# A blocked causal attention and two MLP layers: masks folded into the maximum product, with a copied operand

## What is computed

```python
scores = scale * np.matmul(q, k.transpose(0, 1, 3, 2))
mask = (pos[:, None] // 64) >= (pos[None, :] // 64)
scores = np.where(mask, scores, -1000000000.0)
scores = scores - np.max(scores, axis=-1, keepdims=True)
attn = np.exp(scores)
attn = attn / (np.sum(attn, axis=-1, keepdims=True) + 1e-09)
out = np.matmul(attn, v)
```

## Time and profile before

| | us |
|---|---|
| median of 3 runs | 841.53 (839.37 to 844.37) |
| the profiled execution | 839.87 |
| its span, first to last instruction | 838.0 |
| attention, up to the first MLP product | 236.7 |
| PE busy | 768.6 (92%) |
| DVE busy | 478.2 (57%) |
| ACT busy | 332.3 (40%) |
| POOL busy | 210.2 (25%) |

### The profile page before, as it was taken

How to read it: one execution, slowest core, us unless ns; L and a number is a source line. 1 busy time by engine, 2 the same in 40 slices (tenths; PEclk the granted TensorE clock), 3 DMA queues, 4 the chain that set the end, 5 groups by cost and what they waited for, 6 DMA issues and landing times.

```text
span 838.0 us, 13290 instructions
## 1 busy us (share of the span) xinstructions
PE 768.6 (92%) x4119; PEld 677.7 (81%) x4120; DVE 478.2 (57%) x809; ACT 332.3 (40%) x647; POOL 210.2 (25%) x219
## 2 busy tenths in 40 slices
PE   2989999999999999999999994299999999999993
PEld 1867888788799999999999993278888888888882
DVE  7537777788779484848576456632122483544261
ACT  1435665667563343526161410231211473433250
POOL 5446667666420000000010000212122132122111
PEclk9989999999999999999999997589999999999998
DMA  2665545454210000000100010377110057160000
GB/s 99 227 211 165 142 123 146 141 142 137 66 30 0 1 1 38 1 38 1 39 1 38 1 38 38 124 281 287 38 50 29 25 183 285 38 235 36 14 25 8
DMA packets 50626, 73.79 MB, mean 88 GB/s; under 512 B 28396, under 2 KB 28556, under 8 KB 50576
## 3 DMA queue, kind: packets, MB, share of 16 engines
q1 hardware_dynamic: 46976, 63.71, 23.3%
q0 software_dynamic: 3600, 9.44, 3.1%
HBM read 64.77 MB, written 10.56 MB: 90 GB/s over the span
## 4 chain that ended last, share of the span: by engine, by line
PE 79%; DVE 9%; DMA 5%; SPq 3%; issue 2%; ACT 1%; POOL 1%; POOLq 0%; DVEq 0%
PE ps L687 20%; PE ps L688 19%; PE ps L689 19%; PE ps L640 7%; DMA sums<-o_raw 3%; PE ps L618 3%; PE ps L793 2%; PE ps L677 2%; PE ps L619 2%; PE ps L591 2%; PE ps L766 1%; DVE sig L1126 1%; DMA qk_raw<-qkT 1%; SPq L333 1%; DMA inv_scratch<-sums 1%
## 5 line engine op out<-in xcount | busy, mean ns | idle before, releaser
L640 PE MATMUL ps<-pT,v_sb 128*128 128x320 f32 (+4 forms) x448 | 117.3, 386 | 1.5 <-issue 1.5
L640 PEld LDWEIGHTS ps<-pT,v_sb 128*128 128x128 f32 (+1 forms) x448 | 72.1, 193 | 18.0 <-issue 9.1
L817 ACT ACTIVATE pT<-ps 128x256 f32<-128x256 f32 (+2 forms) x192 | 64.4, 389 | 28.5 <-PE ps L619 25.3
L687 PE MATMUL ps<-we_hi,xgT_hi 128*128 x176 | 72.8, 413 | 2.2 <-DVE xgT_lo L1295 2.2
L687 PE MATMUL ps<-we_hi,hT_hi 128*128 x176 | 71.5, 407 | 2.7 <-DVE hT_lo L1301 2.7
L688 PE MATMUL ps<-we_lo,xgT_hi 128*128 x176 | 70.5, 401 | 0.0
L689 PE MATMUL ps<-we_hi,xgT_lo 128*128 x176 | 70.4, 400 | 0.0
L688 PE MATMUL ps<-we_lo,hT_hi 128*128 x176 | 69.6, 395 | 0.0
L689 PE MATMUL ps<-we_hi,hT_lo 128*128 x176 | 69.6, 395 | 0.0
L687 PE MATMUL ps<-ksq_hi,wm_hi 128*128 128x384 f32 x192 | 65.8, 343 | 1.6 <-DVE yT L1136 1.6
L999 DVE TENSOR_REDUCE negm<-ps 128x1 fp32r<-128x128 f32 (+3 forms) x128 | 57.1, 469 | 15.4 <-PE ps L592 15.1
(11 more groups left out here) (205 smaller groups left out, 1730.1 us busy)
## 6 DMA issues: line engine op xcount, KB each, us to landing
we_raw<-w SPq DMA_DIRECT2D x12, 2048.0 KB, 9.3
qk_raw<-qkT SPq DMA_DIRECT2D x32, 576.0 KB, 4.2
inv<-inv_scratch SPq DMA_DIRECT2D x32, 144.0 KB, 3.0
y_scratch<-ytok SPq DMA_DIRECT2D x6, 768.0 KB, 3.4
v_sb<-v SPq DMA_DIRECT2D x32, 128.0 KB, 3.5
wm_raw<-w_k SPq DMA_DIRECT2D x4, 512.0 KB, 4.5
wm_raw<-w_v SPq DMA_DIRECT2D x4, 512.0 KB, 6.1
wm_raw<-w_r SPq DMA_DIRECT2D x4, 256.0 KB, 4.9
```

The source lines that it names most:

```text
L640: last = mm(ps[:, OUTB + half, q0 - 256 * half:q1 - 256 * half], v_sb[0:rows, j % 2, c, cols], pT[0:rows, i % 2, at + q0:at + q1], start=( ...
L687: mm(dst, a_hi, b_hi, start=(k == 0), stop=False)
L817: return nc.scalar.activation(dst, src, ACT.Exp, **kw)
```

## The change

`q_hi`, `k_both`, `q_lo` and `k_hi` become two tiles a buffer: `hi` (128 rows; q and k) and `aug` (69 rows; three planes, QMAX = 0, QLO = 1, KHI = 2). Rows 0 to 63 of the planes QMAX and KHI are filled by a DMA from `hi` within SBUF (`load_aug`); rows 64 to 68 are written by VectorE once a buffer. The maximum product becomes one product of these 69 rows for each tile, with the mask in rows 65 to 68, and `mask_q` x `mask_k` is gone. For the maximum k's lower half is left out. The subtraction for q goes from GpSimd to VectorE, the cast of q from VectorE to ScalarE, ScalarE's second cast of k is gone. The 1e-9 is added by ScalarE's copy as a bias. Weights come in 20 pieces of 512 columns (256 KB), one a turn in turns 0 to 19. The operands of MLP step 0 are made later: w = 0 in heads 28 to 31 chunk by chunk, w = 1 within step 0, and step 1's w = 1 after step 0's sigmoid. The diff, cut to its core:

```diff
             def load_qk(i):
                 wait(sp, q_split, i - 1)
-                wait(sp, k_is_hi, i - 1)
+                wait(sp, k_split, i - 1)
...
+            def load_aug(i):
+
+                sp.wait_ge(q_is_hi, i + 1)
+                sp.wait_ge(k_is_dup, i + 1)
+                sp.dma_start(aug[i % NBUF][0:DH, QMAX:KHI + 1:KHI - QMAX, 0:S].bitcast(F32),
+                             hi[i % NBUF][0:DH, :, :].bitcast(F32)).then_inc(aug_loaded[i % NBUF], 16)
...
             def load_wm(q):
-                for at, src, n, cols in ((0, wk_in, 1, FF), (WR, wr_in, 1, DM), (WV, wv_in, 2, DM)):
-                    dst = wm_raw[:, at + n * q * cols:at + n * (q + 1) * cols].rearrange("p (c f) -> p c f", c=n)
-                    sp.dma_start(dst, src[:, n * q:n * q + n, :]).then_inc(wmlp_loaded, 16)
...
+                wait(sp, wmlp_loaded[q % WTURN], 16 * (q // WTURN))
+                sp.dma_start(wm_raw[:, q * WLOAD:(q + 1) * WLOAD], src).then_inc(wmlp_loaded[q % WTURN], 16)
...
             load_v(0)
+            load_aug(0)
+            load_aug(1)
             load_qk(2)
             load_row(0)
             load_qk(3)
+            load_aug(2)
...
                 if i % 2 == 0 and i + 2 < NHEAD:
                     load_v(i // 2 + 1)
-                if i < 4:
+                if i < WMLP // WLOAD:
                     load_wm(i)
+                if i + NBUF < NHEAD:
+                    load_aug(i + NBUF)
...
             def head_max(i, groups):
...
-                    pe.wait_ge(q_is_hi, i + 1)
-                    pe.wait_ge(k_split, i + 1)
+                    pe.wait_ge(aug_loaded[i % NBUF], 16 * (i // NBUF) + 16)
...
-                            mm(ps[:, bank, col:col + keys], q_tile, k_both[b][:, 0:keys], start=True, stop=False)
-                            last = mm(ps[:, bank, col + keys - BLK:col + keys], mask_q[:, :], mask_k[:, :],
-                                      start=False, stop=True)
+                            last = mm(ps[:, bank, col:col + keys], q_tile, a[:, KHI, 0:keys], start=True, stop=True)
...
-                        mm(dst, k_both[b][:, keys], q_hi[b][:, q0:q1], start=True, stop=False)
-                        last = mm(dst, k_hi[:, b, keys], q_lo[:, b, q0:q1], start=False, stop=True)
+                        mm(dst, hi[b][:, KEY, keys], hi[b][:, Q, q0:q1], start=True, stop=False)
+                        last = mm(dst, aug[b][:, KHI, keys], aug[b][:, QLO, q0:q1], start=False, stop=True)
...
-                pe.wait_ge(xm_split, 2 * s + 1)
+                if s:
+                    pe.wait_ge(xm_split, 2 * s)
+                else:
+                    pe.wait_ge(xm0_split, DC)
...
-                nc.scalar.activation(o_raw[:, i % NBUF, q0:q1], ps[:, OUTB + half, 0:q1 - q0],
-                                     ACT.Copy).then_inc(o_copied, 1)
+                nc.scalar.activation(o_raw[:, i % NBUF, q0:q1], ps[:, OUTB + half, 0:q1 - q0], ACT.Identity,
+                                     bias=eps[:, i % 2:i % 2 + 1]).then_inc(o_copied, 1)
...
+                nc.scalar.activation(hi[i % NBUF][:, Q, :], qk_raw[:, i % 2, 0, :], ACT.Copy).then_inc(q_is_hi, 1)
...
+                if i in (NHEAD - 4, NHEAD - 2):
+                    for c in range(2):
+                        xm_first(0, 0, c + (i == NHEAD - 2) * 2)
+                if i in (NHEAD - 3, NHEAD - 1):
+                    for c in range(2):
+                        xm0_hi(c + (i == NHEAD - 1) * 2)
             copy_out(NHEAD - 1, 1)
...
-                    if s + 1 < NSTEP:
+                    if s == 0:
+                        xm_first(f // DC, 1 - f // DC, f % DC)
+                    elif s + 1 < NSTEP:
                         xm_first(s + 1, f // DC, f % DC)
+                    if s == 0 and f == DC:
+                        xm_hi(0, 1)
...
+                if s == 0:
+                    for c in range(DC):
+                        xm_first(1, 1, c)
                 if s + 1 < NSTEP:
                     xm_hi(s + 1, 1)
...
-                vec.tensor_scalar_add(sums[:, i % 2, :], sums[:, i % 2, :], 1e-9).then_inc(sums_chain, 1)
...
+            def split_q_lo(i):
+
+                dve.wait_ge(q_is_hi, i + 1)
+                vec.tensor_tensor(aug[i % NBUF][0:DH, QLO, 0:S], qk_raw[0:DH, i % 2, 0, :],
+                                  hi[i % NBUF][0:DH, Q, :].bitcast(F32), ALU.subtract).then_inc(q_split, 1)
...
+            def set_aug(b):
+
+                rows = aug[b][DH:AUG, :, :]
+                vec.memset(rows.bitcast(F32), 0.0).then_inc(aug_made, 1)
...
+            set_aug(0)
+            split_k_hi(0)
+            split_k_hi(1)
+            set_aug(1)
+            split_q_lo(0)
             for g in range(4):
                 head_reduce(0, g)
             copy_row(0)
-            split_hi(2)
+            split_q_lo(1)
+            set_aug(2)
+            split_k_hi(2)
...
-                    if s + 1 < NSTEP:
+                    if s == 0:
+                        sum_xm(f // DC, 1 - f // DC, f % DC)
...
+                    if s == 0 and f == DC:
+                        xm_lo(0, 1)
...
                 else:
+                    for c in range(DC):
+                        sum_xm(1, 1, c)
+                    xm_lo(1, 1)
                     dve.wait_ge(norm_done, NHEAD)
```

More of the change, by code:

```diff
@@ L126, in attention_moe_program @@
         relu_k = place("work", "relu_k", [P, 2, NT])
-        ksq = place("work", "ksq", [P, 2, NT])
-        xsum = [None, None]
-        xsum[1] = place("work", "xsum_r", [P, DC, NT])
+        xsum = [place("work", f"xsum{w}", [P, DC, NT]) for w in range(2)]
         sig = place("work", "sig", [P, DC, NT])
@@ L133, in attention_moe_program @@
         top["work"] = max(top["work"], attention_end)
-        xm[0] = place("work", "xm_k", [P, 2, DC, NT], R32)
-        xsum[0] = place("work", "xsum_k", [P, DC, NT])
+        xm[0][0] = place("work", "xm_k_hi", [P, DC, NT], R32)
+        ksq = place("work", "ksq", [P, 2, NT])
         assert top["work"] <= top["w_mlp"]
@@ L212, in attention_moe_program @@
         WR, WV = DC * FF, DC * FF + DC * DM
+        WLOAD, WTURN = 512, 4
+        assert DM == WLOAD and FF == 2 * WLOAD
         HALF = DC * FF
@@ L853, in _ @@
             for i in range(NBUF):
-                split_k_hi(i)
+                split_q_hi(i)
             def xm_first(s, w, c):
-                wait(act, xm_split, (w, 2, 2 * s + w - 1)[min(s, 2)])
+                if s or w:
+                    wait(act, xm_split, 2 * (s - 1) + w)
+                    dst = xsum[w][:, c, :]
+                else:
+                    wait(act, xm0_split, c - 1)
+                    dst = ksq[:, c % 2, :]
                 for bb, t0, n, at in step_parts(s):
-                    last = nc.scalar.activation(xsum_of(s, w)[:, c, at:at + n], xT[:, DC * bb + c, t0:t0 + n],
-                                                ACT.Copy, scale=omu[:, w, c:c + 1])
+                    last = nc.scalar.activation(dst[:, at:at + n], xT[:, DC * bb + c, t0:t0 + n], ACT.Copy,
+                                                scale=omu[:, w, c:c + 1])
@@ L1043, in _ @@
-            vec.memset(mask_k[0:1, :].bitcast(F32), 1.0).then_inc(const_done, 1)
-            for b in range(NBUF):
-                vec.tensor_copy(q_lo[DH:AUG, b, 0:S], aug[DH:AUG, 0, :])
-                last = vec.tensor_copy(k_hi[DH:AUG, b, :], aug[DH:AUG, 1, :])
-            last.then_inc(aug_made, 1)
-            dve.wait_ge(aug_made, 4)
-            vec.memset(k_hi[DH:DH + 1, :, :].bitcast(F32), 1.0).then_inc(aug_set, 1)
+            vec.tensor_copy(idw[:, 1, PAD:PAD + P], ident[:, :]).then_inc(const_done, 1)
```

195 lines of the change are left out of this document (96 added, 99 removed).

## The result

The kernel after takes 904.67 us (median of 4 runs, 899.35 to 912.08), the kernel before beside it 842.95: a ratio of 1.074 with a 95% interval of 1.065 to 1.083. That is slower, as forecast, but by 7.4% where 3.7 to 3.9% was forecast. The profiled execution is 903.48 us, its span 901.7, which is 63.7 more than the 838.0 before.

A forecast was written before the change was run, and what follows sets the result against it. TensorE (PE), busy 92%, was taken as the bound. Attention +17.7 and -0.5, start -0.5, MLP +6.6 gave +23.3 on 839.87: 863.2; clock falls +9, and the profiled execution's 1.7 under the median, made about 874 us; range 848 to 911.

The forecast's parts named there:

- rival (a): Attention: the clock falls after nearly every wait of PE, 14 x 3.4 us on top of 863, about 911; chance 0.17.
- Part 1: PE in attention: four mask products a head go, 0.48 us a head, 6.22 to 5.74; 13.4 us over 28 heads.
- Part 2, the copy behind v: Turns with v loads: copy issued 6.13 us after the head's scores start, landing at 9.7; loop of two heads 14.3 us.
- Part 2, the turn without v: Copy issued 3.87 us after the head's scores start, landing at 8.3; its 12.9 us loop hides in the 14.3.
- Part 3: Weight pieces ahead of the copy in turns 0 to 19: 0.8 us each, loop of two heads 15.1 us.
- The clock: Attention: 4 falls to 1.2 GHz behind PE's 14 waits for the copy, 2.3 us each, +9 us.
- Part 4: Start of the kernel, mask building replaced by VectorE's mask sets: -0.5 us, between -3 and +2.
- Part 6: First MLP step: operands made later keep PE waiting, +6.6 us in all.
- yT: First MLP step: sums, cast and subtraction for step 1's second operand delay yT, which PE awaits: +4.7 us.
- f = 4: First MLP step, chunk product 4: a cast before ScalarE's square and a subtraction on VectorE delay PE, +1.6 us.
- The transition: Attention to MLP: the last two chunks of xm_k finish after head 31's copy, +0.3 us.

The follow-up runs named there:

- e3: Kernel before with its four mask products a head left out: 837.95 us, ratio 0.9945.
- e14: Kernel after with 18 idle products ahead of the first maximum product of every turn: 901.1 us.
- e15: Kernel after with 18 idle products a turn and its 20 weight pieces asked for in turns 0 to 3, five a turn: 902.8 us.
- e7: Kernel after with its 20 weight pieces asked for in turns 0 to 3, five a turn: 914.3 us.
- e6: Kernel after with 12 idle products ahead of the first maximum product of every turn: 908.9 us.
- e5: Kernel after with the sums and subtraction of MLP step 1's second operand moved behind the first three yT: 898.05 us.
- e17: Kernel after with the copy moved in SyncE's turn to behind sums and qk, ahead of inv, v and the weight piece: 898.9 us.

## Why the prediction was off

The direction held, and so did the cause, waits of PE for the copy. The size failed: 874 was forecast, 904.7 came, which is inside the 848 to 911 and near rival (a), but outside the forecast's own 855 to 890. Two steps of the sum failed: the number of falls, and the round at full clock, above all in the turn without v.

- **Part 1.** Held: 5.1 to 4.65 us from head_max to T, 12.6 us over 28 turns (13.4 forecast); e3 shows the same 0.4 a head, and a head without waits takes 5.80 us for the 5.74.
- **Part 2, the copy behind v.** Held once the pieces are through: in turn 20 T+6.17 and T+9.92 for T+6.13 and T+9.7. In turns 2 to 12 it went out at T+7.9 to T+9.6, later than I had it even with a piece.
- **Part 2, the turn without v.** Failed: "I add nothing for it" and "which it therefore hides in". In turns 1 to 13 its issue was nearly right (T+4.1 to T+4.6 for T+3.87) and its landing wrong, T+9.8 to T+11.0 where I had T+8.3: it made the long wait. From turn 15 on the cast was late, issue T+6.3 to T+8.8, and the copy was hidden only behind a slow or long turn. What the even turns had in the forecast came partly in the odd ones and the other way round; it is luck that the sum is 51 us for the forecast's 46, 47 of them waits for the copy by the view.
- **Part 3.** "I take 0.8" for a piece was too little where it stands in a full queue: it landed 1.5 us behind qk, and the copy 1.2 us behind it (58.63 and 59.85), and the store behind them then stopped the queue. At nearly full clock the pieces are worth 9.0 us over the 24 heads (e14 against e15) for the 5.6 in the forecast, at the clock as it was nothing (e7). With pieces the loops took 17.1 us, and 16.7 without falls (e14), for the forecast's 15.1.
- **The clock.** The step that failed, and by where the time lies the largest: "4 falls: +9". There were 13, and 157.0 - 128.2 = 28.8 us more than forecast without falls lie between head_max and T, 26.1 of them in the 13 stretches with a fall. The price was right, 26.1 / 13 = 2.0 for my 2.3; the number was not. My reason, that the waits lie between a short and a long idle time of the earlier trace rows, was no ground for 4 in 14. Rival (a) had 14 falls and 911. What speaks against it there, that a slow PE fills its next wait, is true as well: e14 has ten falls fewer in the 24 heads, by that price 20 us, and only 6.7 came back, beside idle products that need time themselves; in e6's turns 20 to 28, 6.1 of 10.6 did. So the 28.8 us say where the time lies, not what the falls alone cost.
- **Part 4.** -0.5 forecast, +0.8 measured.
- **Part 6, and the end of attention.** yT and f = 4 held within 0.3 us. The transition was 1.3 short; the fall at the wait for yT, 1.5 us by e5, and the slower head 30 (6.55 us for 5.39, with its wait of 1.4 for ScalarE) were not in the sum. Together 11.2 for 6.6 - 0.5 = 6.1, of which some 0.5 stay unassigned.

In one line, against the profiled executions: 31.3 us were missing (863.2 + 9 is 872.2, not the 872.4 that I wrote), of them 19.8 between head_max and T, nearly all where the clock was low, 5.3 from T to head_max, 5.1 behind turn 29, 1.3 at the start, up to rounding.

A rule of the Trainium skill that I weighed, "DMA: Bandwidth & Descriptors", anatomy of one DMA (about 2.0 us and the bytes over 436 GB/s for a DMA on the GpSimd path), gives 2.7 us for this copy, as an estimate. No run shows less than 3.2, and 3.4 is the median with nothing in front. The Trainium skill, "TensorE: Matmul & The Clock Gate", has the pattern in its section on HAM oscillation: a kernel that waits for a DMA in every tile pays the transition in every tile and not once. This trace agrees, with 13 falls at 13 waits of 2.3 us or more. The same section of the Trainium skill puts the loss at half of the throttled time, by the 61.2 us of the 13 stretches 30.6, as an estimate; the 13 stretches from head_max to T with a fall are 26.1 us longer, and at least 6.7 came back where the falls were taken away.

What stays open is the round's own length at full clock without idle products. It is at most 15.4 us for two heads without pieces (e6, turns 20 to 28) and at most 16.7 with them (e14, turns 6 to 18); no run gives the lower end. So it is open, too, how the missing time divides between falls and round. A fourth buffer, which would let the casts start before the scores end, wasn't tried.

## What to carry to other kernels

Before a DMA is put between two engines, follow the round that it closes: what frees its source, what stands ahead of it in its queue, and what the issuing engine holds back while it waits; here the round was head_max, scores, casts, copy, head_max, and a copy by the engines on the same partitions took the DMA out of it, and 57 us with it. Where a tight PE gets a wait of about 3 us in every second head, count a fall of the clock for each one and not for some, as here 13 at 13, and then subtract what the slow stretch takes off the next wait. After a bottleneck is gone, look for the next DMA in the same queue (here qk) before expecting the whole gain.

## What the runs showed of the hardware

The time of a small DMA depends on the bytes in flight ahead of it far more than the medians of the earlier trace rows let me think: the copy of 288 KB took 3.2 us at best, 3.4 ahead of qk, 4.3 in its place in the kernel after and up to 6.6, 5.9 right behind 576 KB of qk; the sums of 2.2 KB took 1.8 us as a rule and 4.3 at most in e17. In e17 alone the same copy took 5.1 to 6.9 us where it was issued 0.6 us behind qk, and 3.3 to 3.5 where it was issued 2 us or more behind it. I had priced its 288 KB behind another transfer by the difference of two medians, 0.8 us; right behind qk in e17 it landed 1.0 to 1.7 us after it. And idle products are a poor tool for holding the clock in a round that is nearly full: with 12 a head falls remained, with 24 they were the bound, and with 18 they needed 15.6 us of a loop's 16.5 themselves.
